# Attention weighed by groups of four heads, in halves of TensorE's columns, with keys and queries split by ACT and DVE

## The reference

```python
# q, k, v: (2, 8, 768, 64); n_sink 4, window 128
scores = scale * np.matmul(q, k.transpose(0, 1, 3, 2))
keep = is_sink | in_window                     # causal, 128 keys back, or one of the first 4
a = np.exp(np.where(keep, scores, -1e9) - max)
a = a / (np.sum(a, axis=-1, keepdims=True) + 1e-09)
x = np.matmul(a, v)                            # to (1536, 512)
h = np.maximum(x @ w_in, 0.0); x = h * h @ w_out            # 512 -> 2048 -> 512
h = x @ w_in2; g = P(h) / (Q(h) + 1e-6); out = g @ w_out2   # a rational function of h
```

## Time and profile before

| | us |
|---|---|
| median of 3 runs | 671.87 (670.46 to 673.82) |
| profiled execution | 672.72 |
| its span | 670.9 |
| TensorE busy | 654.5 |
| DVE busy | 447.9 |
| ACT busy | 377.7 |
| POOL busy | 330.9 |

### The profile page before, as it was taken

How to read it: one execution, slowest core, us unless ns; L and a number is a source line. 1 busy time by engine, 2 the same in 40 slices (tenths; PEclk the granted TensorE clock), 3 DMA queues, 4 the chain that set the end, 5 groups by cost and what they waited for, 6 DMA issues and landing times.

```text
span 670.9 us, 10181 instructions
## 1 busy us (share of the span) xinstructions
PE 654.5 (98%) x3714; PEld 617.3 (92%) x3714; DVE 447.9 (67%) x665; ACT 377.7 (56%) x804; POOL 330.9 (49%) x316
## 2 busy tenths in 40 slices
PE   7999999999999999999999998999999999999997
PEld 6889998999999999999999997889899999999995
DVE  6656564444344344343466679999899989998995
ACT  3755555334444354443322256677877787778874
POOL 3968573313242212300022337777777767776773
PEclk9999999999999999999999999999999999999999
DMA  7743241203311113100043430002100210001001
GB/s 248 258 146 119 97 162 40 64 1 121 93 40 40 40 40 134 40 9 1 20 125 124 127 110 0 1 1 95 48 1 0 95 48 0 1 1 48 1 0 53
DMA packets 28971, 43.49 MB, mean 65 GB/s; under 512 B 4080, under 2 KB 19440, under 8 KB 28400
## 3 DMA queue, kind: packets, MB, share of 16 engines
q1 hardware_dynamic: 28912, 42.74, 19.6%
HBM read 36.44 MB, written 6.29 MB: 64 GB/s over the span
## 4 chain that ended last, share of the span: by engine, by line
PE 77%; DVE 14%; ACT 3%; issue 3%; POOL 2%; DMA 1%; DVEq 0%; SPq 0%; ACTq 0%; POOLq 0%
PE h_ps L1146 22%; PE y_ps L1158 18%; PE y_ps L1384 15%; PE s_ps L1146 7%; PE o_ps L1233 4%; PE o_ps L1146 3%; DVE s_ps L879 3%; PE s_ps L1216 2%; PE s_ps L1200 2%; DVE o_ps L879 2%; DVE sq L842 2%; DVE p_buf L882 1%; DVE p_buf L873 1%; DVE h_ps L879 1%; DMA y_scratch<-xT 1%
## 5 line engine op out<-in xcount | busy, mean ns | idle before, releaser
L1146 PE MATMUL h_ps<-xT,weights 128*128 128x384 f32 x960 | 190.2, 340 | 0.7 <-ACT sq L594 0.7
L1146 PEld LDWEIGHTS h_ps<-xT,weights 128*128 128x128 f32 x960 | 167.4, 188 | 2.5 <-issue 1.0
L1158 PE MATMUL y_ps<-hid,weights 128*128 128x384 f32 x768 | 156.7, 344 | 0.0
L1384 PE MATMUL y_ps<-weights,hid 128*128 128x512 f32 x576 | 144.3, 395 | 2.3 <-POOL hid L561 1.0
L1158 PEld LDWEIGHTS y_ps<-hid,weights 128*128 128x128 f32 x768 | 134.5, 188 | 0.7 <-issue 0.2
L1384 PEld LDWEIGHTS y_ps<-weights,hid 128*128 128x128 f32 x576 | 107.2, 188 | 24.3 <-POOL hid L561 2.4
L656 ACT ACTIVATE bprobs<-bnegs,neg_max 128x288 f32<-128x288 f32 (+2 forms) x96 | 72.0, 759 | 67.2 <-DVE neg_max L925 66.8
L842 DVE TENSOR_TENSOR sq<-sq 128x384 f32<-128x384 f32 x64 | 45.4, 710 | 88.9 <-ACT sq L594 88.8
L561 POOL TENSOR_TENSOR hid<-p_buf,hid 128x384 fp32r<-128x384 f32 x63 | 64.8, 1028 | 40.0 <-ACT hid L762 39.6
L552 POOL TENSOR_TENSOR q_buf<-h_abs,q_buf 128x384 f32<-128x384 f32 x64 | 64.8, 1013 | 34.5 <-ACT q_buf L617 32.0
L879 DVE RECIPROCAL s_ps<-q_buf 128x384 f32<-128x384 f32 x31 | 79.4, 2561 | 3.2
(11 more groups left out here) (102 smaller groups left out, 940.4 us busy)
## 6 DMA issues: line engine op xcount, KB each, us to landing
weights_raw<-in_w_pack SPq DMA_DIRECT2D x32, 512.0 KB, 4.6
bk_raw<-in_k_pack SPq DMA_DIRECT2D x24, 256.0 KB, 3.3
q_raw<-in_q_pack SPq DMA_DIRECT2D x24, 256.0 KB, 3.4
bv<-in_v_pack SPq DMA_DIRECT2D x24, 128.0 KB, 2.0
y_scratch<-xT SPq DMA_DIRECT2D x2, 1536.0 KB, 6.1
xT<-y_scratch SPq DMA_DIRECT2D x2, 1536.0 KB, 7.2
out_y<-out_stage SPq DMA_DIRECT2D x3, 768.0 KB, 3.5
out_y<-out_stage SPq DMA_DIRECT2D x3, 256.0 KB, 2.9
```

What stands on the lines that cost most here:

```text
L1146: ins = nc.tensor.matmul(bank, weights[:, i, wp, W_IN, t * P:(t + 1) * P], x, start=(t == 0 and n == 0), stop=(t == KC - 1 and n == 2))
L1158: ins = nc.tensor.matmul(y_ps[:, m, 0:NT], weights[:, i, wp, W_OUT, m * P:(m + 1) * P], hid[:, i % 2, gp, :], start=(i == 0 and n == 0), s ...
L1384: ins = nc.tensor.matmul(y_bank(turn, t), hid2[:, i % RING, gp, t * P:(t + 1) * P], weights[:, i, wp, W_OUT, :], start=(i == 0 and n == 0) ...
```

## The change

From unit 30 the slots are replaced by steps over pairs of heads. For pair p (units 2p, 2p+1) step A scores both, into the two banks of `s_ps`, and, where p is odd, weighs a whole group; step B turns units 2p-2 and 2p-1 into the same two banks. A and B go into halves of layer steps in turn. A(p) waits for both copies of B(p-1), and B(p) for both reads of A(p).

Weighing exchanges the operands: 64 columns of `bv` are stationary and 128 queries of `bpT` stream. Even heads are written to partitions 0 to 63 of `o_ps`, odd ones to 64 to 127, so the tile comes out turned, and the products of even and odd heads stand in different halves of the array's columns. Sinks are weighed head by head. The inverse row sums have to be turned now: ACT spreads them over `o_sb` (`spread`), TensorE turns that in an event F, ACT copies it to `inv_cols`, and DVE multiplies (`divide`, event M). The high part follows in the next half (X), the low part in L.

POOL does nothing in this stretch any more. ACT rounds keys and queries (`split_high`), DVE subtracts (`split_low`), and DVE takes the low parts of late weight tiles. `bprobs` is laid out by head, so that exp writes without a stride; the sinks of four heads are packed by one more ACT copy. The lead weighs up to unit 23 instead of 26. The store of the first block's result moves up one group in SP's queue.

The core of the diff:

```diff
-    P_RING = 3
-    N_RING = 4
+    N_RING = 3
+    P_ALL = U_ALL // 2
-        q_raw3 = sb("q_raw3", [P, 3, GROUP * P], F32, band)
+        q_pair = sb("q_pair", [P, 2, GROUP * P], F32, band)
-        bprobs = sb("bprobs", [P, 2, BAND, GROUP], F32, band)
-        bpT = sb("bpT", [P, P_RING, 3 * P], F32, band)
+        bprobs = sb("bprobs", [P, 2, GROUP, BAND], F32, band)
+        bsinks = sb("bsinks", [P, 2, GROUP, SINK_CAP], F32, band)
+        bpT = sb("bpT", [P, (2 * GROUP + 1) * P], F32, band)
+        inv_cols = sb("inv_cols", [P, DM], F32, band)
...
         def score_bank(u):
-            return y_ps[:, 0, :] if u < LEAD and u % 2 else s_ps[:, 0, :]
+            if u < LEAD:
+                return y_ps[:, 0, :] if u % 2 else s_ps[:, 0, :]
+            return s_ps[:, u % 2, :]
...
+        def steps():
+            found = []
+            for p in range(LEAD // 2, P_ALL + 2):
+                qt = p // PAIRS - 1
+                found.append(("A", p))
+                if p % PAIRS == 1:
+                    found += [("M", qt), ("X", qt)]
+                    if qt % QT == QT - 1:
+                        found.append(("L", qt))
+                if p <= P_ALL:
+                    found.append(("B", p))
+                if p % PAIRS == 1 and qt % QT < QT - 1:
+                    found.append(("L", qt))
+                if p % PAIRS == 0:
+                    found.append(("F", qt))
+            return found
...
             def load_q(k):
                 if EARLY + 3 <= k:
-                    sp.wait_ge(kq_ready, k - EARLY - 2)
+                    sp.wait_ge(kq_ready, k - EARLY - 1)
...
@@ POOL @@
-                for blk in range(BLOCKS - 1):
-                    for i in range(FT):
-                        for s, qt in events(blk, i, 0) + events(blk, i, 1):
-                            if s is not None:
-                                slot(s)
-                        if blk == 0 and i + EARLY_W < FT:
-                            weight_low(i + EARLY_W)
...
@@ ACT @@
+                def split_high(k):
+                    act.wait_ge(k_loaded[k % 4], 16 * (k // 4 + 1))
+                    wait_queries(act, k)
+                    act.wait_ge(u_scored, GROUP * (k - 1))
+                    act.wait_ge(kq_ready, k - EARLY)
+                    nc.scalar.activation(bkT[:, heads_of(k), own_cols(k)], bk_raw[:, heads_of(k), own_cols(k)],
+                                         ACT.Copy)
+                    nc.scalar.activation(bq_hi[:, k % 2, :], queries(k), ACT.Copy).then_inc(bq_high, 1)
+                def step(kind, n):
+                    if kind == "A":
+                        if n < P_ALL:
+                            exp(2 * n)
+                        if n % PAIRS == 0:
+                            spread(n // PAIRS - 1)
+                    if kind == "B":
+                        if n < P_ALL:
+                            exp(2 * n + 1)
+                        pT_part(2 * n - 1)
+                        if n < P_ALL and with_sinks(2 * n + 1):
+                            pack_sinks(n // 2)
+                        if n % 2 and EARLY + 2 <= n // 2 + 2 < GROUPS:
+                            split_high(n // 2 + 2)
...
@@ DVE @@
+                def step(kind, n):
+                    if kind == "A":
+                        if n % PAIRS == 0:
+                            sums(n // PAIRS - 1)
+                        if n < P_ALL:
+                            scores(2 * n)
+                            scores(2 * n + 1)
+                        if n % 2 == 0 and EARLY + 2 <= n // 2 + 1 < GROUPS:
+                            split_low(n // 2 + 1)
+                    if kind == "M":
+                        divide(n)
+                    if kind == "B":
+                        pT_part(2 * n - 2)
...
@@ TensorE @@
+                def weigh_group(g):
+                    qt, m, i = unit(GROUP * g)
+                    wait_turned_copies(pe, 2 * g + 1)
+                    pe.wait_ge(bv_loaded[g % 4], 16 * (g // 4 + 1))
+                    if m == 0:
+                        pe.wait_ge(o_read, qt - 1 if qt == QT else qt)
+                    tiles = 1 if i == 0 else 2
+                    for t in range(tiles):
+                        for h in range(m, m + GROUP):
+                            rows, at = slice(D * (h % 2), D * (h % 2) + D), turned_at(h) + t * P
+                            ins = nc.tensor.matmul(o_ps[rows, h // 2 * P:h // 2 * P + P], bv[:, t, D * h:D * (h + 1)],
+                                                   bpT[:, at:at + P], start=(h < 2 and t == 0),
+                                                   stop=(i < 2 and h >= H - 2 and t == tiles - 1),
+                                                   skip_group_check=True)
+                    if i >= 2:
+                        for h in range(m, m + GROUP):
+                            rows = slice(D * (h % 2), D * (h % 2) + D)
+                            ins = nc.tensor.matmul(o_ps[rows, h // 2 * P:h // 2 * P + P], bvs[:, D * h:D * (h + 1)],
+                                                   bpT[:, 2 * GROUP * P:], start=False, stop=(h >= H - 2),
+                                                   skip_group_check=True)
+                    ins.then_inc(u_pv, GROUP)
+                def step(kind, n):
+                    if kind == "A":
+                        if n < P_ALL:
+                            wait_turned_copies(pe, n - 2)
+                            if n % PAIRS == 1:
+                                pe.wait_ge(inv_copied, n // PAIRS - QT)
+                            score(2 * n)
+                            score(2 * n + 1)
+                        if n % 2:
+                            weigh_group((n - 3) // 2)
+                    if kind == "B":
+                        if n < P_ALL:
+                            pe.wait_ge(u_negs, 2 * n + 2)
+                        else:
+                            wait_turned_copies(pe, n - 2)
+                        turn_p(2 * n - 2)
+                        turn_p(2 * n - 1)
+                    if kind == "F":
+                        turn_inv(n)
```

More of the change, by code:

```diff
@@ L693, in banded @@
                         if more:
-                            for s, qt in events(blk, i, 0):
-                                event(s, qt)
+                            for kind, n in events(blk, i, 0):
+                                step(kind, n)
                         if nxt:
@@ L955, in slot @@
                 def slot(s):
-                    if s < U_ALL:
-                        scores(s)
-                    if 2 <= s < U_ALL + 2 and s % 2 == 0:
+                    scores(s)
+                    if s >= 2 and s % 2 == 0:
                         pT_part(s - 2)
@@ L998, in banded @@
                         if more:
-                            for s, qt in events(blk, i, 1):
-                                event(s, qt)
+                            for kind, n in events(blk, i, 1):
+                                step(kind, n)
+                            if blk == 0 and i + EARLY_W < FT:
+                                weight_low(0, i + EARLY_W, w_ready)
                         elif i >= 2:
@@ L1288, in some @@
                             if more:
-                                for s, qt in events(blk, i, half):
-                                    event(s, qt)
+                                for kind, n in events(blk, i, half):
+                                    step(kind, n)
                         if i + 1 < FT:
```

257 lines of the change are left out of this document (160 added, 97 removed).

## The result

| | before | after |
|---|---|---|
| median, same chip | 671.27 (670.46 to 673.82) | 679.54 (676.91 to 681.67) |
| ratio to before, 95% interval | | 1.0115 [1.0067, 1.0162] |
| profiled execution | 672.72 | 680.46 |
| its span | 670.9 | 678.6 |
| lead ends (first layer-1 product) | 44.52 | 46.08 |

The changed kernel is 8 us slower. The spans differ by 7.7: 1.6 in the lead, 5.9 in the stretch with attention, 0.2 behind it. The page of the changed kernel, in the lines that answer to the earlier trace rows: busy time, the chain by engine, and from the strip in 40 slices the granted clock.

A forecast was written before the change was run, and what follows sets the result against it. TensorE, busy 98% of the span, was taken as the bound. The terms -12.5 - 1.8 + 5.4 - 4.1 + 8.8 + 0.5 = -3.7 us took the 671.87 median to 668.2; range 656 to 688.

The forecast's parts named there:

- values stationary: Weighing in the attention stretch: 384 half-width records take 23 us instead of 35.5, -12.5 (from -14.4 to +6.7).
- changes of the array's form: TensorE around each group's weighing: 36 changes between whole array and halves at 0.15 us each, +5.4 (0 to 12.6).
- waits that go: TensorE's waits for neg_max, xT and o_sb in the attention stretch vanish, 3.6 us plus restarts: -4.1.
- lead: Before the first layer-1 product: weighing of units 24 to 26 (1.35) and a 0.4 wait go, -1.8 us.
- keys and queries: They land late in the attention stretch; ACT waits to split them, delaying its ReLU and TensorE: +8.8 us (0 to 14).
- part 5: Waits that come in the attention stretch: late keys and queries +8.8, first-block copies +0.5, SP's other queue edits 0.
- DVE's layer subtractions at 0.56 throughout: Sign in the attention stretch: DVE's 384-column subtractions take 0.56 us, not the 2.07 seen beside POOL's subtraction.
- more than eight: Sign against the prediction: it is wrong if waits stand in more than eight places.
- (a): Rival, weighing: halves don't run beside each other or products don't use half arrays, 42.2 for 23, +19.2, 687; chance 0.20.
- (b): Rival, attention stretch: ACT's lateness never reaches TensorE and mode changes cost nothing, 654 us; chance 0.15.
- (c): Rival, hand-over of the two score banks: one 1 us wait in half of 33 pairs, +16, 684; chance 0.10.
- The forecast's case: Whole kernel: the summed terms hold, 668.2 us for the median, range 660 to 676; chance 0.50.

The follow-up runs named there:

- doubling: Kernel with keys and queries issued ahead of values, every weighing product of the pair steps done twice: 686.0 us, ratio 1.0193 to the kernel before.
- values last: Changed kernel, from group 10 on SP issues a group's values behind the next group's keys and queries: 664.6 us, ratio 0.9884; in a second comparison 664.5, 0.9854.
- The first experiment: Changed kernel with first-layer weight tiles 11 to 15 issued one group earlier in SP's queue: 674.4 us against 672.2 before, ratio 1.0030.
- the parts: Values last kernel, each group's weighing cut into first tile, second tile and sinks with a layer product between: 674.35 us, against 664.5 uncut.
- the kernel built to be (a): Values last kernel with every weighing product written to the lower 64 partitions: 687.2 us against 673.45 for the kernel before, ratio 1.0201.
- the second experiment: The values last kernel: changed kernel with keys and queries issued ahead of the previous group's values from group 10 on, 664.6 us, ratio 0.9884.

## Why the prediction was wrong

It said 668.2, faster at 0.46; it is 679.5. The range held it and the direction was wrong. By its steps:

| step | forecast | measured | from |
|---|---|---|---|
| values stationary | -12.5 | -14.5 | 21.0 (doubling) - 35.5 |
| changes of the array's form | +5.4 | +6.2 | 27.2 in place - 21.0 |
| waits that go | -4.1 | +0.2 | 4.3 before, 4.5 with values last |
| no row for it | | -1.0 | stretch 266.7, and the lines above |
| lead | -1.8 | -0.8 | 43.70 for 44.52 |
| keys and queries | +8.8 | +10.6 | stretches 277.2, 266.6 |
| copies in the first block | +0.5 | in "waits that go" | |
| the late weight tile in SP's queue | 0 | +4.5 | stretches 281.7, 277.2 |
| rest of the lead, half clock above all | not there | +2.4 | 46.08 for 43.70 |
| sum | -3.7 | +7.6 | span +7.7 |

**The step that failed is the path of part 5: it followed two of the loads behind the gate, and the rest of SP's queue was put at 0.** I followed keys and queries through SP's queue, and found where they stand behind a gated load. I didn't follow the late weight tiles, which stand in the same queue behind the same gate. Neither their place nor the engine that rounds them was changed. The gate was: with a whole group weighed in one place it opens one layer step later, 0.2 us ahead of ACT's turn instead of 8.6, and the tile needs 6.3. The first experiment shows it: one edit of the order, and the 6.0 of ACT and the 4.2 of TensorE are gone. With it the measured time is 1.003 of before, and that is within 0.5%. It is not faster, as was forecast; for that the second step that failed is needed, the waits that go.

**The clock was not in the sum.** The forecast priced each wait at its length and 0.1 of restart. The 4.16 was followed by 5.8 us at 0.50, worth 2.6; in the lead of this execution a wait of 1.34 at 15.4 was followed by a stretch at 0.50. The window of the changed kernel's lead, columns as above:

```profile
16.00:20.00 4.00, 3.59 (x13) 2.60 (x12) 2.57 (x11) 1.85 (x7) 3.57 (x3) 0.50 0.80 314
```

In the two versions without that fall the lead ends at 43.46 and 43.70. The records from 15.44 to 21.50 took 5.65 without their wait, and 3.04 in the first experiment: 2.6 by the clock. Then 1.1 more goes to a wait of 1.59 for o_sb at 43.40, where the others have 0.5, and other waits of the lead are shorter by as much. The mean clock of this execution was 0.989, and 0.994 to 0.997 in the three others of the same kernel, which took 676.9 to 681.7. They have no trace, so how much of the 2.4 is in the median isn't shown. The version with all heads in the lower half, whose lead is that of the version with the values last, shows the same fall in its lead and ends it at 45.61; so it comes in some executions and not in others.

**The lead (-1.8).** 0.8 was found. The 12 records and the wait of 0.42 are gone, and two waits of 0.50 stand at its end that weren't there, for o_sb at 41.02 and for xT at 43.70. Leads of one and the same kernel end as far apart as 43.07 and 44.59 (low parts on POOL), so a term of 1 us can't be told here.

**Waits that go (-4.1).** The step was right in what it removed: neither TensorE's wait of 0.98 for xT nor those of 0.73 are there with the values last. It was wrong in its name. It asked what goes and not what is late next. Four waits of 0.48 to 1.07 come in the first block, and the two largest stand behind DVE's new work. With the values last:

```profile
53.43 2.08 DVE L938 TENSOR_TENSOR hid<-sq,hid 128x384 fp32r<-128x384 f32 x1 [0.59 <-ACT hid L632]
...
56.22 1.43 DVE L953 TENSOR_TENSOR weights<-weights_raw,weights 128x1024 fp32r<-128x1024 f32 x1 [0.37 <-ACT weights L672]
57.57 1.26 DVE L1032 TENSOR_SCALAR row_den<-row_sum 128x8 f32<-128x8 f32 x1
```

DVE's subtraction of 384 columns takes 2.08 there while POOL's weight subtraction runs (52.52 to 55.10), so the sign "DVE's layer subtractions at 0.56 throughout" failed; the row sums take 1.26 beside POOL's last split, and between the two DVE's own weight subtraction of 1.43 stands ahead of the score reads. TensorE waits 0.98 at 55.90 and 1.07 at 59.88. The forecast had 0.5 for all of this.

**Keys and queries (+8.8).** Right in mechanism, place and size. The order of steps gave pairs 18, 20, 22, 24, 28 and 40 (the transposes behind B(17), B(19) and so on), at 1.2 or 1.6 with their restart; the first experiment shows waits at just these six, 0.97 to 1.44. The 10.6 holds, beside them, a ReLU wait and a fall of the clock; without these two it is 8.6. The family stands in seven places in the changed kernel and in eight in the first experiment, so "more than eight" didn't come true for it; counted over all kinds TensorE waits in 15 places of the stretch.

**Values stationary, and the array's form.** Together -7.1 was forecast. From rows, a full group costs 1.65 in place: 0.92 and 0.54 for its records, 0.09 ahead, 0.10 in the six products behind. 14 full groups, two of 16 records at 1.23 and two of 8 at 0.80 make 27.2, against 35.5: -8.3. With the values last the whole stretch is 9.1 shorter though its waits are 0.2 longer. The 1 us over may be what the waits of before cost beyond their listed length (1.9, above); that isn't shown. Of the 27.2, 21.0 are records (doubling), which leaves 6.2 for 18 times in and out: 0.34 each, as the parts show by themselves.

Here the pages of the Trainium skill were weighed. TensorEngine Tiling (Array Packing), Key Properties, says that a change of the tiling mode drains TensorE. The traces fit it: going in and out costs 0.34. The Trainium skill's TensorE: Matmul & The Clock Gate, Part 3, has 2.38 times for three column tiles; an estimate from it was 26.5 us for these records. Here two halves gave 0.1125 / 0.055 = 2.0 times, and the measurement decides.

**The rivals.** (a) didn't hold: 0.058 a record, and the kernel built to be (a) took 687. (b), 654, had the lateness at zero and the changes of form at zero. With the lateness gone the time was 664.5: 654 and the 6.2 of the changes and the 4.1 of waits that came back are 664. That it comes out so closely is in part luck, since the smaller differences of the table cancel. (c) didn't hold, by the second experiment. The forecast's case, with "waits that go" at zero, would have been 668.2 + 4.1 = 672.3; the first experiment, which lacks only the late tile, took 674.4.

## What to carry to other kernels

When a change moves the event that opens a gated transfer, list everything that stands behind it in the queue, also what the change doesn't touch, and compare for each when it will land with when its user comes to it. When a step moves from an idle engine to a busy one, do this for its operands above all: an idle engine hides a late landing, a busy one in fixed order hands it on. Repair the order of the queue before judging such a change: one edit of SP's order turned 1.0115 into 0.985 and 0.988. To price a switch of the array's form, repeat the switch and divide, since the gap ahead of it shows only a part.

## What the runs showed of the hardware

- Products in different halves of the array's columns run beside each other in both orders that were tried: 0.058 a record of 128 columns, first ones included, and 0.1125 when all are in one half.
- Going into halves and out again costs 0.34 us behind layer products of 384 columns, paid in the last record of either side.
- TensorE went on at half its pace behind waits of 4.16, 3.55 and 1.36 us, and not behind others of 1.44 and 1.45 us. At one and the same place (pair 16) the granted clock stayed at 1.00 behind a wait of 2.41 in the doubled version and fell to a mean of 0.66 over 4 us behind one of 2.42 with all heads in the lower half. So the length of the wait doesn't decide it; what does no run here shows.
- Exp without a stride in its output took 0.53 us for 288 columns, where it took 0.814 with a stride of four:

```profile
L685 ACT ACTIVATE bprobs<-bnegs,neg_max 128x288 f32<-128x288 f32 x52 | 27.5, 529 | 33.3 <-DVE neg_max L1011 33.1
```

The function and the input are the same, so the layout of the output is what differs. It isn't POOL's idleness: with the splits back on POOL the same exps take 0.529 too. It was off TensorE's path, and no run here was made to see it in the time.
